# Attention with cluster masks on one Trainium2 core: key numbers spread by a repeated stationary column, and the rank product on GpSimd

## What is computed

```python
B, H, S, D = 2, 8, 768, 64          # 16 heads (b, h) of 768 tokens; 16 clusters
q_assign = argmax(einsum('bhsd,hcd->bhsc', q_n, c_n), axis=-1)
k_assign = argmax(einsum('bhsd,hcd->bhsc', k_n, c_n), axis=-1)
mask = q_assign[:, :, :, None] == k_assign[:, :, None, :]
scores = where(mask, scale * q @ k.T, -1e9)
attn = exp(scores - max(scores)); attn /= attn.sum(-1) + 1e-9
out = attn @ v
...
x = routed_experts(out); return dense_mixture(x)
```

## Time and profile before

| | before |
|---|---|
| median of 3 runs | 1625.68 us |
| the profiled execution, its own time | 1627.19 us |
| its span | 1625.40 us |
| TensorE busy | 1587.3 us (98%) |
| VectorE busy | 1202.6 us (74%) |
| ScalarE busy | 775.5 us (48%) |
| GpSimd busy | 257.9 us (16%) |

### The profile page before, as it was taken

One profiled execution on the slowest core, in us unless ns is written; L12 is line 12 of the kernel. 1 busy time (PEld: TensorE's weight loads), 2 busy tenths in 40 slices (PEclk: granted clock), 3 DMA queues, 4 the chain that ended last, 5 costly groups with the idle time before them and its releaser, 6 DMA issues.

```text
span 1625.4 us, 26973 instructions
## 1 busy us (share of the span) xinstructions
PE 1587.3 (98%) x8352; PEld 1396.8 (86%) x8352; DVE 1202.6 (74%) x2025; ACT 775.5 (48%) x1377; POOL 257.9 (16%) x299
## 2 busy tenths in 40 slices
PE   9999999889999989999999999999999999999998
PEld 7888888767777767989989899898999989899897
DVE  7999999999999994777666656566666666656664
ACT  5777778778888862333232332323323233332321
POOL 2111111113433250010010001001000100100102
PEclk7999999999999999999999999999999999999999
DMA  4222233243633401011011001001100100110002
GB/s 99 59 59 58 58 74 99 65 146 124 225 123 128 143 26 40 27 40 39 27 37 41 26 26 52 26 26 39 39 26 26 52 26 26 41 36 26 26 0 78
DMA packets 123699, 94.91 MB, mean 58 GB/s; under 512 B 66344, under 2 KB 101160, under 8 KB 123632
## 3 DMA queue, kind: packets, MB, share of 16 engines
q1 hardware_dynamic: 120848, 86.01, 17.5%
q0 software_dynamic: 2480, 8.13, 1.7%
q10 hardware_dynamic: 304, 0.05, 0.0%
HBM read 87.88 MB, written 6.29 MB: 58 GB/s over the span
## 4 chain that ended last, share of the span: by engine, by line
PE 83%; DVE 10%; issue 4%; ACT 1%; DVEq 1%; DMA 0%; SPq 0%; POOL 0%; ACTq 0%
PE moe_bank L1332 11%; PE moe_bank L1330 11%; PE moe_bank L1331 11%; PE moe_bank L1307 10%; PE moe_bank L1310 10%; PE moe_bank L1309 10%; DVE attn_probs_t_lo L628 2%; PE moe_bank L1253 2%; PE moe_bank L1255 2%; PE moe_bank L1254 2%; DVE attn_scores L680 2%; PE moe_bank L1266 2%; PE moe_bank L1268 2%; PE moe_bank L1267 2%; PE attn_ps_probs_t L419 2%
## 5 line engine op out<-in xcount | busy, mean ns | idle before, releaser
L1954 DVE SCALAR_TENSOR_TENSOR all_x<-moe_bank,all_x 128x512 f32<-128x512 f32 x336 | 251.3, 748 | 129.7 <-PE moe_bank L1332 127.7
L1307 PE MATMUL moe_bank<-moe_x_t_hi,all_w_hi 128*128 128x384 f32 x896 | 304.5, 340 | 3.0 <-DVE all_w_lo L870 2.9
L1310 PE MATMUL moe_bank<-moe_x_t_hi,all_w_lo 128*128 128x384 f32 x896 | 302.4, 338 | 0.0
L1309 PE MATMUL moe_bank<-moe_x_t_lo,all_w_hi 128*128 128x384 f32 x896 | 301.6, 337 | 0.0
L1330 PE MATMUL moe_bank<-moe_w_hi,moe_h_hi 128*128 128x512 f32 x768 | 301.1, 392 | 0.2 <-DVE moe_w_lo L870 0.2
L1331 PE MATMUL moe_bank<-moe_w_lo,moe_h_hi 128*128 128x512 f32 x768 | 300.7, 392 | 0.0
L1332 PE MATMUL moe_bank<-moe_w_hi,moe_h_lo 128*128 128x512 f32 x672 | 265.0, 394 | 0.0
L1307 PEld LDWEIGHTS moe_bank<-moe_x_t_hi,all_w_hi 128*128 128x128 f32 x896 | 168.2, 188 | 14.0 <-issue 3.6
L1309 PEld LDWEIGHTS moe_bank<-moe_x_t_lo,all_w_hi 128*128 128x128 f32 x896 | 168.1, 188 | 11.3
L1310 PEld LDWEIGHTS moe_bank<-moe_x_t_hi,all_w_lo 128*128 128x128 f32 x896 | 168.0, 187 | 0.0
L1331 PEld LDWEIGHTS moe_bank<-moe_w_lo,moe_h_hi 128*128 128x128 f32 x768 | 144.2, 188 | 22.4
(11 more groups left out here) (324 smaller groups left out, 3096.8 us busy)
## 6 DMA issues: line engine op xcount, KB each, us to landing
all_w_raw<-in_moe_w SPq DMA_DIRECT2D x8, 2048.0 KB, 7.6
moe_w_raw<-in_moe_w SPq DMA_DIRECT2D x8, 2048.0 KB, 9.6
moe_dense_w_raw<-in_moe_w SPq DMA_DIRECT2D x64, 256.0 KB, 2.9
moe_dense_w_raw<-in_moe_w SPq DMA_DIRECT2D x32, 512.0 KB, 3.3
attn_q_raw<-in_q SPq DMA_DIRECT2D x32, 192.0 KB, 3.3
attn_k_raw<-in_k SPq DMA_DIRECT2D x32, 192.0 KB, 3.8
attn_v_raw<-in_v SPq DMA_DIRECT2D x16, 192.0 KB, 3.8
tokens<-all_x SPq DMA_DIRECT2D x32, 96.0 KB, 2.0
```

What stands on the lines that cost most here:

```text
L1307: pe.matmul(out, hi[:, s, k, :], XH[chunk][:, x, k, :], start=(start and k == 0), stop=False, skip_group_check=True)
L1309: pe.matmul(out, hi[:, s, k, :], XL[chunk][:, x, k, :], start=False, stop=False, skip_group_check=True)
L1310: mm = pe.matmul(out, lo[:, s, k, :], XH[chunk][:, x, k, :], start=False, stop=(stop and k == 1), skip_group_check=True)
L1954: dve.scalar_tensor_tensor(acc, y, PROB[:, row, bass.ds(at, 1)], acc, ALU.mult, ALU.add).then_inc(y_added, 1)
```

## The change

The rank product (L656) leaves VectorE's chain for GpSimd, except for head 0. The last maximum (L659) is no longer issued at the end of the step with t = 0, but in the next step, behind its maxima and ahead of its mask; it waits for GpSimd's product through a new semaphore `ranked`. The diagonal is gone: GpSimd copies the six columns of key numbers to bf16, and TensorE takes each of the six as a stationary matrix, one column repeated 128 times, and multiplies it with the identity, 128 columns at a time. For head 0 VectorE makes that copy.

```diff
-        DIAG = mem.sbuf("key_id_diagonal", [P, T, P], BF16)
+        IDB = mem.sbuf("key_id_b", [P, T], BF16)
...
             def key_ids(out, first):
-                pe.matmul(out[:, 0:3 * P], c["onesb"][:], DIAG[:, first:first + 3, :].rearrange("p n k -> p (n k)"),
-                          start=True, stop=True).then_inc(prep_ready, 1)
+                for n in range(first, first + 3):
+                    mm = pe.matmul(out[:, (n - first) * P:(n - first + 1) * P], IDB[:, n:n + 1].broadcast_to([P, P]),
+                                   c["identb"][:], start=True, stop=True)
+                mm.then_inc(prep_ready, 1)
...
                                       ALU.is_ge).then_inc(ids_step, 1)
-                    dve.wait_ge(ids_step, 4 * g + 2)
-                    dve.tensor_tensor(SIM[:], SIM[:], c["rank16"][:].rearrange("p (o c) -> p o c", o=1).broadcast_to([P, 2 * T, NC]),
-                                      ALU.mult).then_inc(ids_step, 1)
-                    dve.wait_ge(ids_step, 4 * g + 3)
-                    dve.tensor_reduce(ID[j][:], SIM[:], AX.X, ALU.max).then_inc(ids_step, 1)
+                    if isinstance(g, int) and g == 0:
+                        rank(dve, ranked)
+                        numbers(g, j)
+
+            def numbers(g, j):
+                dve.wait_ge(ranked, g + 1)
+                dve.tensor_reduce(ID[j][:], SIM[:], AX.X, ALU.max).then_inc(ids_step, 1)
...
                 if not isinstance(n, int) or n + 2 < G * T:
                     maxima(n + 2, s + 2)
+                if s % T == 1 and (not isinstance(i, int) or 2 * i + s // T + 1 < G):
+                    numbers(2 * i + s // T + 1, (s // T + 1) % 2)
                 if not isinstance(n, int) or n + 3 < G * T:
                     mask(n + 3, s + 3, 2 * i + (s + 3) // T)
...
-            dve.wait_ge(ids_step, 4)
-            dve.tensor_tensor(DIAG[:], c["identb"][:].rearrange("p (o k) -> p o k", o=1).broadcast_to([P, T, P]),
-                              ID[0][:, T:2 * T].rearrange("p (m o) -> p m o", o=1).broadcast_to([P, T, P]),
-                              ALU.mult).then_inc(diag_ready, 1)
+            dve.wait_ge(ids_step, 3)
+            dve.tensor_copy(IDB[:], ID[0][:, T:2 * T]).then_inc(idb_ready, 1)
...
-            def diagonal(g, j):
-                pool.wait_ge(ids_step, 4 * (g + 1))
+            def key_numbers(g, j):
+                pool.wait_ge(ids_step, 3 * g + 2)
+                pool.sem_inc(passed_pool, 1)
+                pool.tensor_tensor(SIM[:], SIM[:], c["rank16"][:].rearrange("p (o c) -> p o c", o=1).broadcast_to([P, 2 * T, NC]),
+                                   ALU.mult).then_inc(ranked, 1)
+                pool.wait_ge(ids_step, 3 * (g + 1))
                 if not isinstance(g, int) or g > 0:
                     pool.wait_ge(prep_ready, 6 * g)
-                pool.tensor_tensor(DIAG[:], c["identb"][:].rearrange("p (o k) -> p o k", o=1).broadcast_to([P, T, P]),
-                                   ID[j][:, T:2 * T].rearrange("p (m o) -> p m o", o=1).broadcast_to([P, T, P]),
-                                   ALU.mult).then_inc(diag_ready, 1)
+                pool.sem_inc(passed_pool, 1)
+                pool.tensor_copy(IDB[:], ID[j][:, T:2 * T]).then_inc(idb_ready, 1)
```

More of the change, by code:

```diff
@@ L242, in attention @@
         pair_cleared, pair_ready = mem.sem("cents_of_pair_cleared"), mem.sem("cents_of_pair_ready")
-        diag_ready = mem.sem("diag_ready")
+        idb_ready = mem.sem("key_id_b_ready")
+        ranked = mem.sem("sims_ranked")
         kid_ready = mem.sem("kid_ready")
@@ L393, in prep @@
                 elif stage == 5:
-                    pe.wait_ge(diag_ready, g + 1)
+                    pe.wait_ge(idb_ready, g + 1)
                     key_ids(ps_p[:], 0)
@@ L505, in tensor @@
             scores(0, 0, 0)
-            pe.wait_ge(diag_ready, 1)
+            pe.wait_ge(idb_ready, 1)
             key_ids(ps_t[:, 0], 0)
@@ L624, in scalar, with rank @@
             copy_out_t(G // 2 - 1, 13)
+        def rank(engine, done):
+            engine.wait_ge(ids_step, 2)
+            engine.tensor_tensor(SIM[:], SIM[:], c["rank16"][:].rearrange("p (o c) -> p o c", o=1).broadcast_to([P, 2 * T, NC]),
+                                 ALU.mult).then_inc(done, 1)
         def vector(dve, experts):
@@ L650, in prep @@
                     dve.tensor_reduce(SMX[:].rearrange("p (a b) -> p a b", a=4), sims, AX.X, ALU.max).then_inc(ids_step, 1)
-                    dve.wait_ge(ids_step, 4 * g + 1)
+                    dve.wait_ge(ids_step, 3 * g + 1)
                     dve.tensor_tensor(SIM[:].rearrange("p (a b) c -> p a b c", a=4), sims,
@@ L829, in step @@
                     if t == 0:
-                        diagonal(g + 1, j_next)
+                        key_numbers(g + 1, j_next)
                     if t == 3:
```

## The result

| | before | after |
|---|---|---|
| median of the runs | 1625.56 us (4 runs, 1625.21 to 1625.98) | 1613.88 us (4 runs, 1612.91 to 1614.62) |
| the profiled execution, its own time | 1627.19 us | 1614.62 us |
| its span | 1625.40 us | 1612.8 us |

The ratio is 0.9922 (95% interval 0.9904 to 0.9939): 11.7 us faster. Forecast were 1617.1 us, with a range of 1610.5 to 1623.0. In a second comparison, with its own runs of before, the ratio was 0.9926 (0.9909 to 0.9942).

What follows compares the result with a forecast made beforehand. VectorE sets the attention stage's pace, TensorE close behind. Six short heads at 0.27 us and eight long at 0.98, less 0.3, give -9.2; the start's +0.6 makes -8.6, forecasting 1617.1 us (range 1610.5 to 1623).

Steps and rivals of the forecast that it cites:

- clean overlap: Rival: GpSimd's V subtraction meets neither the denominator's sum nor a mask; 1610.8 us, chance 0.15.
- rival on TensorE: Rival: TensorE, also waiting for ScalarE's copy of the first key numbers, lets only half VectorE's gain through; 1624.8 us, chance 0.12.
- (a): VectorE's chain: the rank product leaves it, -0.39 us per head.
- (b): VectorE: the chain's last maximum moves behind the next maxima; at most 0.1 us per head may close, taken as 0.
- (c): GpSimd forms the rank product in 610 ns, hidden beside VectorE's maxima with next to nothing to spare; taken as 0.
- (d): GpSimd's diagonal becomes a six-column copy: VectorE's mask stall goes, -0.33 us per head; TensorE's 0.27 wait goes.
- (e): TensorE's key numbers: two matmuls of 384 columns become six of 128, +0.44 us per head, hidden in its slack.
- (f): GpSimd's V subtraction against VectorE: long heads lose a 0.71 us stall, both kinds get a new mask stall of 0.45.
- (g): The start, where TensorE is the chain at half speed: key-number matmuls cost +0.4 us, second head +0.2; together +0.6.
- Late product: Rival: GpSimd's product takes 1.0 us and VectorE waits 0.4 us for it in 14 heads; 1622.7 us, chance 0.13.
- TensorE takes over: Rival: TensorE's slack is not free to spend, so only half of VectorE's gain comes out; 1624.8 us, chance 0.12.
- Slow column: Rival: TensorE reads the repeated stationary column slowly, each key-number matmul taking 0.44 us; 1642 us, chance 0.08.

Runs made afterwards that it cites:

- f1: The kernel before, with GpSimd's V subtraction made to wait until the second mask behind the chain is done; 1621.83 us, ratio 0.9975.
- e3: The changed kernel, with GpSimd's V subtraction made to wait for the mask that it held; 1613.30 us, ratio 0.9920 to before.
- e8: The changed kernel with two edits: V subtraction waits for the mask, and fold goes ahead of the second half of key numbers; 1608.61 us.
- e7: The changed kernel, with GpSimd forming the rank product twice, first into a spare tile, so the one that counts comes later; 1616.60 us.
- e1: The kernel before with only the key numbers' spreading changed (GpSimd copy, repeated column on TensorE); chain and rank product stay on VectorE; 1620.55 us.
- e2: The changed kernel with GpSimd's diagonal and the matrix of ones kept, so only rank product and last maximum move; 1622.81 us.
- e5: The changed kernel, with TensorE's fold put ahead of the second half of the key numbers; 1614.17 us, ratio 0.9928 to before.

## Why the prediction was right, and which step failed

**The bound.** Right for before: VectorE's stalls set the kinds of heads (f1), and TensorE's waits for it are all but gone in after. Of after the prediction said that TensorE allows the gain, "in the long kind just so". That is how it came out: with all of VectorE's mask stalls gone, e3 gained only 0.3 us more in the stretch. The clean overlap, one of the rivals (1610.8 us), would have been cut off at 18.0 us per head by TensorE; e3 is that case, built, and took 1613.30, and e8 shows which of TensorE's waits cut it off, the one for ScalarE's copy. The rival on TensorE had named that wait: it did not cost any of the forecast gain, but it is what ends it.

**(a), (b).** The chain of the earlier trace rows starts with

```profile
103.37 0.35 DVE L650 TENSOR_REDUCE attn_sim_max<-attn_ps_prep 128x12 f32<-128x192 f32 x1
```

From there to the maxima were 1.64 us before (to 105.01), and are 0.86 after (98.07 to 98.93); L670 in its new place adds 0.27 (99.81 to 100.08). That saves 0.51, where 0.39 was taken and up to 0.1 more was named for (b): VectorE's last maximum, between two instructions that don't depend on it, costs 0.27, not the 0.47 of the chain.

**(c).** Estimated 0.61 us, measured 0.60; hidden, as forecast, with 0.2 us of margin. e7 shows the price of missing it: the short heads pay, the long ones don't.

**(d).** Right: mask 0.41, numbers on TensorE without a wait for them. The stall was worth 0.44 us (from 0.77 between the starts of mask and low parts to 0.33), 0.33 had been called the least.

**(e).** Estimated at 0.44 us per head and hidden. The six loads of a head take 0.34 us together (twice 0.17), where the two of before take 0.10 each, and the busy time of TensorE's loads rose by 0.10 and 0.20 us per head (16.58 to 16.68, 16.43 to 16.63). So the term was over twice too large. In the steady heads it is hidden, on the edge.

**(f).** Right in mechanism and in sum, by two errors that cancel. VectorE reaches L707 3.27 us behind the start of the chain where it took 4.22 (103.37 to 107.59): a lead of 0.95, not 0.72. So the next mask meets the subtraction earlier: the stall is 1.15 - 0.41 = 0.74 in one kind and 0.64 in the other, not 0.45. From the start of the chain to this mask's end the short kind gains 0.22 and the long kind 1.03 us, and the whole heads 0.31 and 1.03 (18.43 to 18.12, 19.03 to 18.00), against 0.27 and 0.98. That the sum fits so well is in part luck.

**(g), the step that failed.** It had +0.6 us, "the first head +0.4, the second +0.2", and said of VectorE's shorter work there that it "frees nothing". In the chain that ended last of after the first key-number matmuls stand with

```profile
18.66 0.35 PE attn_ps_probs_t L373 x3
19.00 0.32 PE attn_ps_prep L373 x3
```

nearly the 0.34 and 0.32 us of the two single ones before, at half clock in both: six of 128 columns cost what two of 384 did, +0 and not +0.4. And the second head gained 1.8 to 2.3 us instead of losing 0.2, because there TensorE waits for VectorE, whose work in its way became shorter. The second trace of before, in which the similarities' matmuls follow each other every 0.11 us from 26 us on as in after (every 0.21 at half clock), has it:

```profile
27.00 0.36 DVE L650 TENSOR_REDUCE attn_sim_max<-attn_ps_prep 128x12 f32<-128x192 f32 x1 [0.69 <-PE attn_ps_prep L366]
...
28.99 0.96 DVE L680 CUSTOM_DVE_ANT_0 attn_scores<-attn_ps_scores,attn_mask 128x768 f32<-128x768 f32 x1 [0.46 <-issue]
...
29.87 1.20 DVE L668 TENSOR_SCALAR attn_mask<-attn_key_id_rows,attn_cluster_id 128x768 bf16<-128x768 bf16 x1
```
```profile
31.68 0.92 PE L419 MATMUL attn_ps_probs_t<-all_ident,attn_probs 128*128 128x128 f32 x6 [1.21 <-DVE attn_probs_t_lo L628]
```

and after, at the same place:

```profile
27.19 0.36 DVE L659 TENSOR_REDUCE attn_sim_max<-attn_ps_prep 128x12 f32<-128x192 f32 x1 [1.12 <-PE attn_ps_prep L367]
...
27.96 0.96 DVE L691 CUSTOM_DVE_ANT_0 attn_scores<-attn_ps_scores,attn_mask 128x768 f32<-128x768 f32 x1
...
29.11 0.41 DVE L679 TENSOR_SCALAR attn_mask<-attn_key_id_rows,attn_cluster_id 128x768 bf16<-128x768 bf16 x1
```
```profile
30.14 0.92 PE L422 MATMUL attn_ps_probs_t<-all_ident,attn_probs 128*128 128x128 f32 x6
```

From the second maximum (27.00 and 27.19) to TensorE's next transposes it takes 4.68 us before (to 31.68) and 2.95 after (to 30.14). Of the 1.73 us, 1.22 lie ahead of the scores' maxima (1.99 to 0.77): the two instructions that left the chain, and 0.46 us for which VectorE was idle behind it and whose cause the trace does not show. Another 0.5 lies at the mask, which is not held any more (0.8 us less, and 0.3 for L670 in its new place). e1 and e2 each show about half of the whole. The prediction had looked at the chain, seen a TensorE matmul in it, and priced only that matmul. With (g) at -1.8 in place of +0.6 its sum would have been -11.0, against 11.7 measured; of the rest, 0.3 is the 13 heads' 9.5 for 9.2.

The first head's own length is left out of this, since it moves with the granted clock: in 24 to 28 us the traces of before were granted 0.50 (1.2 GHz throughout) and 0.85, those of after 0.74 and 1.00, and in all four TensorE had been busy throughout from 12 to 24 us. From the first to the second maximum that makes 13.05 and 12.14 us before and 12.37 and 11.28 after. In the first trace of before the 0.50 lasts until 32 us, and its second head is 19.09 long, not 18.58. Whether the change has a part in the clock is open: the values of before differ with no edit between them, and the ten traces of the experiments lie between 11.17 and 12.16.

**The rivals.** Late product: not in after. e7's 0.29 us of wait per head cost 2.3 us of the stretch and 0.4 of the second head, and only the short heads and the last paid it; the rival's 5.6 us had 0.4 us paid in all 14. TensorE takes over: its wait for ScalarE's copy came, but not its price. Slow column: refuted, 0.17 us for three loads. One figure beside the sum is slightly off: the 2.9 us over 14 heads are 14 times the 0.19 us between 106.93 and 106.74, which is 2.7.

## What to carry to other kernels

Once two engines are both full, a cut on one of them is worth only the distance to the other, and edits that each give nothing can give 5 us together (e3, e5, e8): before dropping an edit, look whether its wait moved to the other engine, and try the pair. What a GpSimd instruction cost VectorE here went not by its length but by which VectorE instruction it met; a wait in GpSimd's queue, which puts it behind the instruction that it would hold, removed the meeting, at no cost that the runs show (e3, f1). Where the instruction that holds is tied to a third engine, a delay ahead of the held one is hidden in its stall (the long heads of e7). Cost the first pass through a pipeline on its own, by who waits for whom there: the steady heads' slack says nothing of it.

## What the runs showed of the hardware

- VectorE's `tensor_scalar` is held by more than GpSimd's two-input instructions: by the cast of 384 columns (e1, L698 until 0.02 us behind the cast's end) and by a memset, which only writes. The memset is in e2, where no other GpSimd instruction runs beside the mask (the diagonal ends at 29.29):

```profile
29.23 0.85 POOL L832 MEMSET attn_cents_of_pair<- 128x896 f32 x1
```
```profile
29.67 0.62 DVE L677 TENSOR_SCALAR attn_mask<-attn_key_id_rows,attn_cluster_id 128x768 bf16<-128x768 bf16 x1
```

  The mask takes 0.62 us for 0.41 and ends at 30.29, 0.21 behind the memset. Whether the casts of 64 columns hold the sum on three columns is not shown: in after L707 starts at 101.34, beside casts of 101.20 and 101.37 (0.24 us each), and takes its 0.16, but it ends 0.06 behind the first cast's end, later than a held one would.
- How long the held one lasts beyond the holder differs with its size: 0.21 to 0.22 us for the mask of 768 columns (about half of its 0.41), 0.02 to 0.03 for three columns. The Trainium skill, page "SBUF — State Buffer", section "Who interferes with whom", has the second fully blocked while the first one runs, which would put the mask's end at 103.21 + 0.41 = 103.62 in the timeline above; it was 103.43. So the rule is right for who is held, and 0.2 us too dear for this mask, the same as in before.
- It works the other way round too: in e1 the mask at 101.09 takes 0.49 us beside three casts of 64 columns, and the last of these, begun at 101.31 while the mask runs, takes 0.37 us; in after the same cast takes 0.24 to 0.27.
- The scores' maxima, a custom instruction that reads PSUM and SBUF, were not lengthened by the product beside them (0.96 us).
